# The later part of the turned probabilities made by VectorE from PSUM, the turned k copied by ScalarE, GpSimd's weight pieces two steps later

## The reference

```
scores = (q @ k.T) / sqrt(64) + slope_h * -|i - j|    where 0 <= i - j < 128, else -1e9
attn   = exp(scores - max) / (sum + 1e-9)
x      = (attn @ v), as (2304, 512)
logits = x @ w_gate;  expert = argmax;  gate = softmax(logits)[expert]
kept   = the first `capacity` tokens of each expert, in order
out    = gate * (relu(x @ w1[expert]) @ w2[expert])    for kept tokens, else 0
```

## Time and profile before

| | us |
|---|---|
| median of 3 runs (419.81 to 422.93) | 420.14 |
| the profiled execution | 422.48 |
| its span | 420.8 |
| TensorE busy in it | 400.0 (95%) |
| VectorE busy | 254.0 (60%) |
| ScalarE busy | 200.3 (48%) |
| GpSimd busy | 148.9 (35%) |

### The profile page before, as it was taken

How to read it: one execution, slowest core, us unless ns; L and a number is a source line. 1 busy time by engine, 2 the same in 40 slices (tenths; PEclk the granted TensorE clock), 3 DMA queues, 4 the chain that set the end, 5 groups by cost and what they waited for, 6 DMA issues and landing times.

```text
span 420.8 us, 10614 instructions
## 1 busy us (share of the span) xinstructions
PE 400.0 (95%) x2622; PEld 327.5 (78%) x2623; DVE 254.0 (60%) x802; ACT 200.3 (48%) x530; POOL 148.9 (35%) x228
## 2 busy tenths in 40 slices
PE   6969999999989999999999999999999999999981
PEld 5757888887878677788888888888888888888871
DVE  5646767698987678656676335627655567323220
ACT  1847787877667625543345153305554334111110
POOL 7547898825642433122222222211223211122210
PEclk9899999999999999999999999999999999999997
DMA  9998999995410113676666417605656760111100
GB/s 159 195 298 203 245 253 247 266 239 130 103 51 27 50 28 100 227 250 223 205 186 213 167 50 243 224 25 161 197 194 214 238 223 25 50 50 39 50 25 16
DMA packets 80971, 64.08 MB, mean 152 GB/s; under 512 B 63726, under 2 KB 63726, under 8 KB 80944
## 3 DMA queue, kind: packets, MB, share of 16 engines
q1 hardware_dynamic: 73600, 52.19, 46.2%
q0 software_dynamic: 3520, 10.76, 7.9%
q10 hardware_dynamic: 3824, 0.80, 1.1%
HBM read 54.29 MB, written 10.23 MB: 153 GB/s over the span
## 4 chain that ended last, share of the span: by engine, by line
PE 82%; SPq 4%; DVE 4%; issue 3%; POOL 2%; DMA 1%; ACT 1%; DVEq 0%; POOLq 0%
PE ps L1423 54%; PE ps L1285 6%; PE ps L1258 6%; PE ps L1443 4%; SPq L360 4%; PE ps L1296 3%; PE ps L1230 3%; PE ps L1266 3%; PE ps L1416 2%; DMA raw<-in_moe_w 1%; DVE weights_sb L1162 1%; POOL probsT L587 1%; DVE ps L871 1%; DVE probs L884 1%; PE ps L1342 0%
## 5 line engine op out<-in xcount | busy, mean ns | idle before, releaser
L1423 PE MATMUL ps<-weights_sb,rowsT_hi 128*128 (+1 forms) x336 | 107.8, 402 | 0.9 <-DVE weights_sb L1162 0.9
L1423 PE MATMUL ps<-weights_sb,hiddenT_hi 128*128 x320 | 98.6, 389 | 1.2 <-DVE hiddenT_lo L1142 1.2
L809 ACT ACTIVATE hidden<-ps 128x512 f32<-128x512 f32 x20 | 11.9, 597 | 142.3 <-PE ps L1423 142.3
L1162 DVE TENSOR_TENSOR weights_sb<-raw,weights_sb 128x1024 f32 (+1 forms) x56 | 67.2, 1221 | 15.4 <-issue 13.1
L1423 PEld LDWEIGHTS ps<-weights_sb,rowsT_hi 128*128 128x128 f32 x336 | 61.1, 188 | 14.8 <-issue 1.5
L646 POOL DMA_INDIRECT out<-y_sb,dst_now x20 | 20.2, 1008 | 148.1 <-DVE y_sb L1169 148.1
L1423 PEld LDWEIGHTS ps<-weights_sb,hiddenT_hi 128*128 128x128 f32 x320 | 60.0, 188 | 14.1 <-issue 1.4
L1423 PE MATMUL ps<-weights_sb,rowsT_lo 128*128 (+1 forms) x168 | 66.2, 394 | 0.0
L1423 PE MATMUL ps<-weights_sb,hiddenT_lo 128*128 x160 | 62.4, 390 | 0.0
L1142 DVE TENSOR_TENSOR hiddenT_lo<-ps,hiddenT_hi 128x512 fp32r<-128x512 f32 x40 | 25.8, 687 | 58.1 <-ACT hiddenT_hi L813 58.1
L798 ACT ACTIVATE weights_sb<-raw 128x1024 f32 (+1 forms) x56 | 56.6, 1067 | 0.0
(11 more groups left out here) (177 smaller groups left out, 615.1 us busy)
## 6 DMA issues: line engine op xcount, KB each, us to landing
raw<-in_moe_w SPq DMA_DIRECT2D x64, 512.0 KB, 4.4
q_rows<-in_q SPq DMA_DIRECT2D x16, 256.0 KB, 5.8
v_rows<-in_v SPq DMA_DIRECT2D x16, 256.0 KB, 6.2
x_rows<-x_sb SPq DMA_DIRECT2D x16, 256.0 KB, 4.3
k_rows<-in_k SPq DMA_DIRECT2D x14, 256.0 KB, 6.4
k_rows<-in_k ACTq DMA_DIRECT2D x2, 256.0 KB, 7.2
v_rows<-in_v SPq DMA_DIRECT2D x4, 128.0 KB, 5.6
v_front<-in_v SPq DMA_DIRECT2D x4, 128.0 KB, 6.4
```

The source lines that it names most:

```text
L1162: vec.tensor_tensor(weights_sb[:, slot, 2 * layer + 1, part].rearrange("p s n -> p (s n)"), raw[:, j, :], weights_sb[:, slot, 2 * layer, p ...
L1423: ins = te.matmul(dst, left[a], right[c], start=first and n == 0, stop=last and n == 2)
```

## The change

- `keep_later` moves from GpSimd to VectorE. It is now the product of the turned probabilities in PSUM with a mask `laterT` of zeros and ones, which GpSimd makes once. It still waits until ScalarE's copy of them is done. It stands first in each step from kk = 2 on.
- The copy of the turned k moves from VectorE to ScalarE (but for the first two units, whose copies stay on VectorE).
- GpSimd takes weight piece n at step n + 4 instead of n + 2, behind `v_step`, and SP reloads `raw` one unit later. `gather_first` stands ahead of `v_step` in kk = 11 instead of behind kk = 10.
- The beginning: ScalarE copies the first turned q before it waits for `eye_wg` and issues the gate weights; VectorE waits for one mask instead of two, and makes the second four `bias_front` tables behind the first k copy; TensorE has four filler transposes ahead of `turn_k(0, 0)` and four ahead of `score(0, 0)`, and the fillers write another bank.
- `second_layer` takes the products with the upper part of four chunks first (eight matmuls), and waits for the lower part only ahead of the four matmuls that need it. TensorE reads the number of tiles before the last nine matmuls of the first layer of tile 1.

```diff
@@ -123,6 +123,7 @@
         later = sb("later", [P, P])
+        laterT = sb("laterT", [P, P])
         mins = sb("mins", [P, 2, QUAD])
@@ -464,7 +465,7 @@
                 for layer in range(2):
-                    j = u - 1 - CHUNKS * layer
+                    j = u - 2 - CHUNKS * layer
                     if 0 <= j < CHUNKS:
@@ -521,6 +522,10 @@
+            link(g.memset(laterT[:, :], 0.0))
+            g.affine_select(out=laterT[:, :], in_=laterT[:, :], compare_op=ALU.is_ge, fill=1.0, base=0,
+                            pattern=[[1, P]], channel_multiplier=-1).then_inc(masks_done, 1)
+
             for t, first, step in ((iota_e, 0, 1), (iota_eE, E, 1), (iota_t, 0, 1), (iota_p, 0, 1), (iota_key, 0, P)):
@@ -581,12 +586,6 @@
-            def keep_later(b, kk):
-
-                pool.wait_ge(probsT_whole, b * STEPS + kk + 1)
-                g.affine_select(out=probsT[:, 1, :, :], in_=probsT[:, 0, :, :], compare_op=ALU.is_gt, fill=0.0,
-                                base=0, pattern=[[0, QUAD], [-1, P]], channel_multiplier=1).then_inc(probsT_later, 1)
-
             def place_in_columns(n, lo, hi):
@@ -605,16 +604,14 @@
                     u = b * TI + kk // 2
-                    if kk >= 2:
-                        keep_later(b, kk)
+                    if b == 1 and kk == FIRST_INVERTED + 1:
+                        gather_first()
                     if kk % 2 == 1 and u + 1 < UNITS and (u + 1) % TI > 0:
                         step_v(u + 1)
-                    if b == 0 and kk >= 2:
-                        split_weights(kk - 2)
+                    if 0 <= b * STEPS + kk - 4 < 4 * CHUNKS:
+                        split_weights(b * STEPS + kk - 4)
                     if b == 1 and 5 <= kk < FIRST_ROUTED[1]:
                         place_in_columns(0, 2 * (kk - 5), GROUPS[0][1] if kk == 8 else 2 * (kk - 4))
-                    if b == 1 and kk == FIRST_INVERTED:
-                        gather_first()
             place_in_columns(1, *GROUPS[1])
@@ -703,6 +700,12 @@
+            def turned_k(b, i):
+                act.wait_ge(k_turned, b * TI + i + 1)
+                at = HALF + P * place[i]
+                nc.scalar.activation(kT[:, :, at:at + P] if i > 0 else kT_joint[:, :, :],
+                                     turn_ps.rearrange("p (c s) -> p c s", c=DC), ACT.Copy).then_inc(kT_ready, 1)
+
             def copy_mix(b, kk):
@@ -732,8 +735,8 @@
                         copy_mix(b + (kk - 1) // STEPS, (kk - 1) % STEPS)
-                    if quad == 0 and not (last and i + 2 >= TI):
-                        turned_q(b + (i + 2) // TI, (i + 2) % TI)
+                    if not (last and i + 2 >= TI):
+                        (turned_q if quad == 0 else turned_k)(b + (i + 2) // TI, (i + 2) % TI)
                     if last and kk == STEPS - 4:
@@ -759,12 +762,12 @@
             nc.scalar.activation(mins[:, 0, 0:1], ident[:, 0:1], ACT.Exp)
+            turned_q(0, 0)
             act.wait_ge(eye_ready, 1)
...
             act.dma_start(cap_raw[:, :], capacity.broadcast_to([P, 2])).then_inc(wg_landed, 16)
-            turned_q(0, 0)
             turned_q(0, 1, ps[:, 5, :])
@@ -888,7 +891,13 @@
-            def turned_k(b, i, bank=turn_ps):
+            def keep_later(b, kk):
+                dve.wait_ge(probsT_whole, b * STEPS + kk + 1)
+                vec.tensor_tensor(probsT[:, 1, :, :], probsT_ps.rearrange("p (n s) -> p n s", n=QUAD),
+                                  laterT[:, :].unsqueeze(1).broadcast_to([P, QUAD, P]), ALU.mult
+                                  ).then_inc(probsT_later, 1)
+
+            def turned_k(b, i, bank):
                 dve.wait_ge(k_turned, b * TI + i + 1)
@@ -993,8 +1002,8 @@
                     lo, hi = GROUPS[n]
-                    if quad == 1 and not (last and i + 2 >= TI):
-                        turned_k(b + (i + 2) // TI, (i + 2) % TI)
+                    if i > 0:
+                        keep_later(b, kk)
                     if quad == 1:
@@ -1015,6 +1024,8 @@
                     if not (last and kk + 2 >= STEPS):
+                        if first and kk == 1:
+                            dve.wait_ge(masks_done, 4)
                         if first and kk == 2:
@@ -1055,7 +1066,7 @@
             link(vec.memset(eps[:, :], 1e-9))
-            dve.wait_ge(masks_done, 2)
+            dve.wait_ge(masks_done, 1)
             for h in range(H):
@@ -1065,12 +1076,18 @@
             dve.wait_ge(distance_ready, 1)
-            for h in range(H):
-                last = vec.scalar_tensor_tensor(out=bias_front[:, h, :], in0=distance[:, :],
-                                                scalar=2.0 ** (-8.0 * (h + 1) / H), in1=mask_front[:, :],
-                                                op0=ALU.mult, op1=ALU.add)
-            link(last)
+
+            def make_front(quad):
+                for n in range(QUAD):
+                    h = head(quad, n)
+                    last = vec.scalar_tensor_tensor(out=bias_front[:, h, :], in0=distance[:, :],
+                                                    scalar=2.0 ** (-8.0 * (h + 1) / H), in1=mask_front[:, :],
+                                                    op0=ALU.mult, op1=ALU.add)
+                link(last)
+
+            make_front(0)
             turned_k(0, 0, probsT_ps)
+            make_front(1)
             for odd in range(2):
@@ -1398,11 +1415,13 @@
                 for _ in range(n):
-                    te.transpose(turn_ps[:, 0:P], ident[:, :], ident[:, :])
+                    te.transpose(ps[:, 6, 0:P], ident[:, :], ident[:, :])
...
             turn_q(0, 0)
+            fill_early(4)
             turn_k(0, 0, probsT_ps)
+            fill_early(4)
             score(0, 0)
@@ -1447,11 +1466,17 @@
                 pe.wait_ge(y_ready, t + 1)
-                for c in range(FC):
-                    if c % 4 == 0:
-                        pe.wait_ge(hiddenT_ready, t * 2 + c // 4 + 1)
-                    last = product(y_ps(j), [part[:, c, :] for part in hiddenT],
-                                   [weights(slot, kind, D * c, D) for kind in (2, 3)], c == 0, c == FC - 1)
+                for half in range(2):
+                    chunks = range(4 * half, 4 * half + 4)
+                    pe.wait_ge(hiddenT_hi, t * 2 + half + 1)
+                    for c in chunks:
+                        for kind in (2, 3):
+                            te.matmul(y_ps(j), hiddenT[0][:, c, :], weights(slot, kind, D * c, D),
+                                      start=(c == 0 and kind == 2), stop=False)
+                    pe.wait_ge(hiddenT_ready, t * 2 + half + 1)
+                    for c in chunks:
+                        last = te.matmul(y_ps(j), hiddenT[1][:, c, :], weights(slot, 2, D * c, D),
+                                         start=False, stop=(c == FC - 1))
                 last.then_inc(y_done, 1)
@@ -1510,10 +1535,10 @@
             turn_rows(1, 1, 16)
+            pe.wait_ge(tables_ready, 1)
+            tiles = pe.value_load(tiles_to_i[0:1, E - 1:E], min_val=1, max_val=TILES)
             first_layer_chunks(1, 0, slice(0, 1), range(1, DC)).then_inc(hidden_done, 1)
             pe.wait_ge(first_y_ready, 1)
-            pe.wait_ge(tables_ready, 1)
-            tiles = pe.value_load(tiles_to_i[0:1, E - 1:E], min_val=1, max_val=TILES)
             with pe.Fori(0, PAIRS) as pair:
```

## The result

The changed kernel takes 417.74 us in the median of 7 runs (416.47 to 418.43), the kernel before 420.14 (419.81 to 422.93, also 7). The ratio, estimated over all their runs, is 0.9921, with a 95% interval of 0.9892 to 0.995: 3.3 us faster, with an interval of 2.1 to 4.5. The medians alone differ by 2.4. The forecast was 416.2, its range 412.8 to 420.2. Two executions, one of 564.14 us at a mean granted clock of 0.655 (`e5`) and one of 999.98 us (`e7`), are left out of all the times and ratios; no trace shows their cause.

A forecast was written before the change was run, and what follows sets the result against it. TensorE, busy 400 of 420.8 us, was taken to bound the kernel, so only its gaps could shrink. The terms, 5.3 + 0.5 - 0.7 - 1.8 - 0.7 + 0.9 + 0.4 = 3.9 off, turn 420.14 into 416.2 us, range 412.8 to 420.2.

The forecast's parts named there:

- main case: The forecast's own account of the whole change: 3.9 us off, with 2.5 to 5.5 around it, chance 0.50.
- Term 1: Fourth and fifth step, batch 0: later weight pieces remove TensorE's stall behind the raw weights; 5.3 us off, bounds 3.5 to 5.3.
- rival (d): Gap at 29.01 us only changes its owner, another load or `v_step` being late instead: 421 to 422 us, chance 0.04.
- Term 2: Beginning: first steps come forward, limited by the q rows' load for kk = 2; 0.5 us off, bounds 0 to 0.5.
- Term 3: Attention steps: VectorE's `keep_later` delays the minimum that `turn_back` needs; 0.07 in ten odd steps, 0.7 us lost.
- Term 4: Odd steps, mainly batch 0: GpSimd holds VectorE's `sums_eps` through shared ports; 0.45 in four steps, 1.8 us lost.
- Term 5: Routing steps of batch 1: gather stall goes, but `own_ranks`, `first_slot` and their chains queue behind `keep_later`; 0.7 us lost.
- Term 6: Expert tiles: last second layer waits less (0.9) and the register load comes earlier (0.4); 1.3 us off.
- (b): Stall at 29.01 only half returned and port waits at their upper bound: 418 to 420 us, chance 0.18.
- (a): The new order costs VectorE nothing, no delay or port wait in the steps: 6.8 us off, 413.3 us, chance 0.20.
- (c): Slower: GpSimd holds the sums in all 13 odd steps with a `keep_later`, 8.3 us lost, 422.7 us; chance 0.08.

The follow-up runs named there:

- e5: The changed kernel run once more, with nothing altered: 417.56 us, ratio 0.9916 to the kernel before.
- e7: Changed kernel with `keep_later` back on GpSimd, the k copy back on VectorE, and no addition of 1e-9 to the sums: 413.23 us, ratio 0.9818.
- e2: Kernel before with only the weight pieces two steps later (raw reloaded one unit later): 417.83 us, ratio 0.9912.
- e8: Kernel before with only the edits of the beginning: 422.03 us, ratio 1.0009.
- e4: Changed kernel without the instruction that adds 1e-9 to the sums; the reciprocal reads the sums: 415.98 us, ratio 0.9872.
- e6: Changed kernel with the sums and their reciprocal ahead of `keep_later`: 415.79 us, ratio 0.9881.
- e9: Changed kernel with `keep_later` on VectorE and the k copy on ScalarE in batch 0 only, undone in batch 1: 416.06 us, ratio 0.9889.
- e11: Kernel before with only the new order of `second_layer` and the earlier register load: 418.85 us, ratio 0.9958.
- e12: Changed kernel with `keep_later` back on GpSimd, k copy on VectorE, and 1e-9 added as a scalar instead of from a tile: 414.37 us, ratio 0.985.
- e10: Changed kernel with `keep_later` on VectorE and k copy on ScalarE in batch 0 only, without adding 1e-9: 413.54 us, ratio 0.9813.
- e1: Kernel before with only `keep_later` moved to VectorE and the turned k copy to ScalarE: 421.13 us, ratio 0.9985.
- e3: Changed kernel with `keep_later` back on GpSimd, k copy on VectorE, and the gather behind `v_step` of kk = 11: 414.31 us, ratio 0.9831.

## Why the prediction was right, and where not

The time (417.74 for 416.2) and the direction are right, most mechanisms too. The forecast took 3.9 off; the ratio gives 3.3, the medians 2.4, a little under the 2.5 to 5.5 of its main case. The 0.8% lies within 1%, the case that it gave 0.53.

That the sum came so near is partly luck. Between the two profiled executions the terms make 5.9 off, 2.0 more than forecast, as the losses of terms 3 and 4 were smaller and the gains of 2 and 6 larger. Against that stands a 5.3 read from one execution and put onto a median, for which experiment gives 3.7. The two errors have opposite signs. What the runs correct:

| term | forecast | in the two profiles | by experiment |
|---|---|---|---|
| 1 weights later | 5.3 off | 5.27 off | `e2`: 3.7 off |
| 2 beginning | 0.5 off | 1.0 off | `e8`: 0 alone |
| 3 VectorE each step | 0.7 lost | 0.35 lost, 0.07 in five steps | `e4`, `e6`: gone |
| 4 port waits | 1.8 lost | 0.7 lost (`e5`: 2.2) | `e4`: with term 3, 1.8 |
| 5 routing steps | 0.7 lost | 1.0 lost | `e9`: 1.1 back |
| 6 expert tiles | 1.3 off | 1.66 off | `e11`: 1.8 off |

**Term 1** was 5.27 in the profile (kk = 5 starts 6.28 earlier, of which 1.01 came in with the beginning), but the forecast took one execution for the kernel. By `e2` it is worth 3.7 (2.3 to 5.1), near its lower bound of 3.5; the reason given for that bound, weights that land earlier without the profiler, is not one that a trace can show. The stall is 1.9 in `e11` and 6.4 in `e8`. The raw weights land at much the same time (GpSimd's first cast starts at 26.32 before, at 25.93 in `e8` and 25.59 in `e11`), so what the stall costs depends on when TensorE gets there and on whether its clock falls behind it. That this is what makes the spread of the kernel before is argued and not shown. Of its 17 executions in the group of `e11`, the ten with a mean granted clock of 0.987 or more took 419.72 to 421.26 us, the seven with less 421.75 to 423.03. But the mean does not tell the stall by itself: the profiled execution of `e11`, the one with the short stall, has 0.984, as its clock was low at the start, and with 418.66 us it is one of the faster ones of its kernel. The profiled execution of before (0.986) lies 2.3 above its median and the profiled one of after 1.2 below its own, which with the 2.4 between the medians makes the 5.9. Nothing that TensorE needed was late next (it is busy for the whole of 25 to 35 us, at 1.00), so rival (d) is out.

**Term 2** was limited by a load that lands "5.9 later, at 18.2". It was issued at 12.0 and landed 5.6 later; kk = 2 waited 0.15 for it and started at 17.69. What the term left out is the clock. The kernel before and the changed one by stretches, one each:

```profile
10.00:12.00 2.00, 2.00 (x11) 1.67 (x11) 0.96 (x9) 0.91 (x3) 2.00 (x10) 0.50 1.44 151
```

```profile
10.00:12.00 2.00, 1.12 (x13) 0.87 (x12) 1.72 (x11) 2.00 (x10) 1.85 (x10) 1.00 1.41 166
```

Before, TensorE waits 0.90 and 1.36 us with only the four transposes of k between, and then runs at a granted clock of 0.50 (1.2 GHz). In the changed kernel four fillers stand ahead of the first wait (0.91) and four behind the transposes of k, the second wait is 0.51, and the clock stays at 1.00 (2.4 GHz). All ten profiles with the edits of the beginning have 1.00 from 8 to 14 us and start kk = 2 at 17.3 to 18.4; the four without them have 0.50 from 10 to 12 and start it at 18.65 to 19.83. Whether it is the fillers or the shorter second wait (k is copied sooner) no run tells, as the two come together. And the term is worth its 1.0 only together with term 1 (`e8`): ahead of a wait for a load an earlier start is given back. The sum, which adds them, holds because both edits are in it.

**Term 3** is right to the hundredth for one step: in kk = 3 the minimum starts 3.94 behind the step's start (forecast 3.95), and the next step takes 3.68. But it occurs in five steps of batch 0, not in ten, as batch 1 has other waits. **Term 4** has its mechanism right: in all traces together each of the 33 additions that started within a GpSimd subtraction or cast was held to its end. Its size of 1.8 lies between those of the two profiles of the changed kernel (0.6 and 0.1; 1.0, 0.75 and 0.4, by the steps' lengths). Its reason was incomplete: "Both operands of it lie in SBUF" is true, but is not the condition (`e12`). As for the phase, GpSimd is clear of the sums as forecast in kk = 7 and 13 (by 0.83 and 0.68 us), and idle at them in 3 and 17. The late load that it names was there, `v_front` for unit 5: GpSimd waited 5.46 us for it, until 42.88, and the piece behind it met the sums at 45.32. In both profiles GpSimd stands at the sums in four odd steps of batch 0 (kk = 5, 9, 11 and 15), as many as the forecast took, but whether the sums are held is a matter of hundredths. In the first profile those of kk = 11 start just ahead of GpSimd's next instruction:

```profile
52.94 0.16 DVE L909 TENSOR_TENSOR sums_eps<-sums,eps 128x8 f32<-128x8 f32 x1
52.97 1.28 POOL L585 TENSOR_TENSOR weights_sb<-raw,weights_sb 128x512 fp32r<-128x512 f32 x1
```

In `e5` the same sums start at 52.95, in the middle of that instruction, and take 0.84. So the size of the term is in part chance.

**Term 5** came out as 1.0 lost between the starts of batch 1 and of the first tile. In kk = 10 to 12, 0.6 is gained (forecast 0.7), 1.45 of it at kk = 11 where the gather was; in kk = 3 to 7 it is even (0.4 lost); from kk = 13 on 1.7 are lost (1.0). What the sum hides is larger: the exchange costs batch 1 1.9 us (66.18 less 64.25 in the table), which the gather's new place, an edit that doesn't need the exchange, pays back in part. **Term 6** took the register load at 0.4 in bounds of 0 to 0.9; it gave the 0.90 whole. The last tile gave 0.73 in bounds of 0.6 to 0.9.

The rivals, and two slips: the sum of (b) comes to 0.1 lost, not "0.1 off" (the range's 420.2 has it right), and half of the forecast case and all of (a) are 0.45, not 0.43. (a), the exchange costs nothing, is what `e10` shows for batch 0 once no sum can be held, at 413.5; in the changed kernel it did not hold. (b)'s half returned stall is half true, of the kernel before rather than of the change. (c) needed a hold in every odd step; two or three occurred.

What the forecast did not ask is whether two parts of the change remove the same thing. The exchange alone removes the gap at 29 (`e1`), the later weight pieces alone remove it as well (`e2`), and together they remove it once. With the gap gone, the exchange had nothing left to give, and cost some 3 us (`e3`).

## What to carry to other kernels

When a change has several parts, ask of each what it gives once the others are in: here two removed the same stall, and the one that cost something could be left out (414.3 instead of 417.7). A stall on a load is worth what it costs in many executions, not in the profiled one: TensorE may arrive earlier or later, and its clock may fall behind the wait or not. Where an engine has no slack, put its instruction that another engine can hold up into the time in which it waits anyway (`e6`), or use an operation that isn't held, where one gives the same number (`e4`; the scalar addition of `e12` is held as well).
